# Moving a fused kernel's weights by 64 bytes, and writing the first group's gate into PSUM

## The reference

```python
for t in range(S):                                   # attention
    kt, vt, rt, wt = (k[:, :, t], v[:, :, t], r[:, :, t], w[:, :, t])
    cur = np.einsum('bhd,bhe->bhde', u[None] * kt, vt)
    y[:, :, t] = np.einsum('bhd,bhde->bhe', rt, state + cur)
    state = wt[:, :, :, None] * state + np.einsum('bhd,bhe->bhde', kt, vt)

h = x @ w_in                                         # first network, 384 -> 2048 -> 384
g = np.where(h >= 1, h, np.where(h <= -1, 0.0, (h + 1) ** 2 / 4))
x = g @ w_out

g = x @ w_gate                                       # second network, 384 -> 1536 -> 384
silu = g * (1.0 / (1.0 + np.exp(-g)))
out = silu * (x @ w_val) @ w_out
```

## Time and profile before

| what | value |
|---|---|
| median of 3 runs | 992.36 us (992.11 to 992.6) |
| the profiled execution | 992.52 us |
| its span, first to last instruction | 990.6 us |
| TensorE, VectorE, ScalarE, GpSimd busy | 972.9, 519.5, 402.3, 163.5 us |
| mean granted clock of TensorE | 0.999 of full speed |

### The profile page before, as it was taken

How to read it: one execution, slowest core, us unless ns; L and a number is a source line. 1 busy time by engine, 2 the same in 40 slices (tenths; PEclk the granted TensorE clock), 3 DMA queues, 4 the chain that set the end, 5 groups by cost and what they waited for, 6 DMA issues and landing times.

```text
span 990.6 us, 17480 instructions
## 1 busy us (share of the span) xinstructions
PE 972.9 (98%) x6886; PEld 954.7 (96%) x6886; DVE 519.5 (52%) x906; ACT 402.3 (41%) x841; POOL 163.5 (17%) x155
## 2 busy tenths in 40 slices
PE   6999999999999999999999999999999999999998
PEld 5899999999999999999999999999999999999997
DVE  8996666657576575764444433434333343334332
ACT  5665455454554554544665322222222222222222
POOL 6992210301102112020263200000000000000000
PEclk9999999999999999999999999999999999999999
DMA  9724212121222212100332100010100001010000
GB/s 303 238 66 132 85 55 86 53 86 52 87 77 62 87 43 95 68 2 1 132 108 88 57 17 32 1 49 1 48 0 29 19 0 48 0 48 0 24 1 25
DMA packets 23492, 59.52 MB, mean 60 GB/s; under 512 B 2688, under 2 KB 12032, under 8 KB 23424
## 3 DMA queue, kind: packets, MB, share of 16 engines
q1 hardware_dynamic: 23424, 58.59, 18.2%
HBM read 49.14 MB, written 9.44 MB: 59 GB/s over the span
## 4 chain that ended last, share of the span: by engine, by line
PE 94%; DVE 3%; issue 1%; ACT 1%; DMA 0%; DVEq 0%
PE bank L1202 50%; PE bank L1230 35%; PE bank L1258 2%; PE bank L1280 2%; PE bank L1275 1%; PE bank L1250 1%; DVE suf L965 1%; PE bank L1286 1%; PE bank L1267 1%; DVE att L1031 0%; DVE k_r_by_channel L990 0%; DVE k_r_by_channel L987 0%; DMA w_by_channel<-in_w_channel 0%; DVE glo L1055 0%; DVE gate L1062 0%
## 5 line engine op out<-in xcount | busy, mean ns | idle before, releaser
L806 ACT ACTIVATE ghi<-gate 128x384 fp32r<-128x384 f32 x224 | 117.3, 523 | 186.7 <-DVE gate L1074 95.6
L1055 DVE TENSOR_TENSOR glo<-gate,ghi 128x384 fp32r<-128x384 f32 x224 | 133.7, 597 | 113.2 <-ACT ghi L806 111.0
L1072 DVE TENSOR_TENSOR gate<-bank,gate 128x384 f32<-128x384 f32 x96 | 53.5, 557 | 223.2 <-ACT gate L925 223.2
L1202 PE MATMUL bank<-xhi,w2gv_alo 128*128 128x384 f32 x480 | 162.6, 339 | 0.0
L1202 PE MATMUL bank<-xlo,w2gv_ahi 128*128 128x384 f32 x480 | 162.5, 339 | 0.0
L1202 PE MATMUL bank<-xhi,w2gv_ahi 128*128 128x384 f32 x480 | 162.5, 339 | 0.0
L925 ACT ACTIVATE gate<-bank 128x384 f32<-128x384 f32 x96 | 47.3, 493 | 235.8 <-PE bank L1202 235.8
L1230 PE MATMUL bank<-ghi,w1ohi 128*128 128x384 f32 x384 | 134.8, 351 | 2.0 <-DVE ring L1067 1.1
L1202 PE MATMUL bank<-xhi,w1ihi 128*128 128x384 f32 x384 | 130.3, 339 | 1.3 <-issue 0.8
L1062 DVE SCALAR_TENSOR_TENSOR gate<-bank,gate 128x384 f32<-128x384 f32 x128 | 71.1, 555 | 112.4 <-ACT gate L815 112.4
L1230 PE MATMUL bank<-glo,w1ohi 128*128 128x384 f32 x384 | 130.0, 338 | 0.0
(11 more groups left out here) (95 smaller groups left out, 1580.4 us busy)
## 6 DMA issues: line engine op xcount, KB each, us to landing
r_k_v_by_token<-in_rkv_token SPq DMA_DIRECT2D x24, 576.0 KB, 5.0
k_r_by_channel<-in_kr_channel SPq DMA_DIRECT2D x24, 448.0 KB, 4.0
w_by_channel<-in_w_channel SPq DMA_DIRECT2D x24, 226.2 KB, 2.6
x_t<-ring SPq DMA_DIRECT2D x8, 576.0 KB, 2.8
x_raw<-x_t SPq DMA_DIRECT2D x8, 576.0 KB, 4.0
ring<-in_w_out SPq DMA_DIRECT2D x22, 192.0 KB, 2.5
out_t<-ring SPq DMA_DIRECT2D x7, 576.0 KB, 3.1
ring<-in_w_gate SPq DMA_DIRECT2D x12, 192.0 KB, 2.4
```

The costliest lines, as they stand in the source:

```text
L806: e.activation(ghi[j % 2][:, :], gate[j % 2][:, :], ACT.Copy).then_inc(M["hi", ph], 1)
L1055: e.tensor_tensor(glo[j % 2][:, :], gate[j % 2][:, :], ghi[j % 2][:, :].bitcast(F32), ALU.subtract)\
L1072: e.tensor_tensor(q, hid[j % 2][:, 0:T], q, ALU.mult).then_inc(M["t", 2], 1)
L1202: m = e.matmul(out, w_of(a, k), x_of(b_, k), start=start and i == 0, stop=stop and i == total - 1)
```

## The change

Four things. The three small tiles become one of 80 bytes, placed as 96, and the weights begin at 96 bytes beyond a multiple of 256 from xhi (no padding is needed with the sizes at hand); everything behind them moves down by 64 bytes. In group 0 of the first network the gate goes to the PSUM bank of its product instead of to SBUF: VectorE's knee writes there, and ScalarE's hi and VectorE's lo read it there. For that tile_in waits for lo instead of knee, in group 0 from tile 2 on and for the first two tiles of group 1. And in slot 15 of group 0 VectorE does copy_out before the scan.

```diff
+        xhi_at = at[0]
         xhi = [place(f"xhi{i}", [P, KT, T], F32R)[0] for i in range(2)]
...
-        beyond, _ = place("w_beyond", [PR, 2, OPS_CHECK + 2], F32)
-        bad, _ = place("w_bad", [PR, OPS_CHECK + 1], F32)
-        ones, _ = place("ones", [PR, 9], F32)
-        ones = ones[:, 0:1]
+        sums, _ = place("w_sums", [PR, 3 * OPS_CHECK + 2], F32)
+        beyond = sums[:, 0:2 * OPS_CHECK].rearrange("q (b n) -> q b n", b=2)
+        bad, ones = sums[:, 2 * OPS_CHECK:3 * OPS_CHECK + 1], sums[:, 3 * OPS_CHECK + 1:3 * OPS_CHECK + 2]
+
+        W_STEP = 256
+        at[0] += (xhi_at + 96 - at[0]) % W_STEP
...
-        assert w1_at % 64 == 32
...
+        def gate_of(ph, g, j):
+
+            return hid[j % 2][:, 0:T] if ph == 1 and first(g) else gate[j % 2][:, :]
...
-                e.activation(ghi[j % 2][:, :], gate[j % 2][:, :], ACT.Copy).then_inc(M["hi", ph], 1)
+                e.activation(ghi[j % 2][:, :], gate_of(ph, g, j), ACT.Copy).then_inc(M["hi", ph], 1)
...
-                e.tensor_tensor(glo[j % 2][:, :], gate[j % 2][:, :], ghi[j % 2][:, :].bitcast(F32), ALU.subtract)\
+                e.tensor_tensor(glo[j % 2][:, :], gate_of(ph, g, j), ghi[j % 2][:, :].bitcast(F32), ALU.subtract)\
                     .then_inc(M["lo", ph], 1)
...
-                q = gate[j % 2][:, :]
-                e.scalar_tensor_tensor(q, hid[j % 2][:, 0:T], 1.0, q, ALU.max, ALU.min).then_inc(M["g", 1], 1)
+                e.scalar_tensor_tensor(gate_of(1, g, j), hid[j % 2][:, 0:T], 1.0, gate[j % 2][:, :], ALU.max, ALU.min).then_inc(M["g", 1], 1)
...
+                if j == J1 - 1 and first(g):
+                    copy_out(1, g)
                 if after_next:
                     if j in scan_slots(g):
                         scan_window(g + 2, scan_slots(g)[j])
                 if after_next and j == SUM_SLOT:
                     sum_w(g + 2)
-                if j == J1 - 1:
+                if j == J1 - 1 and not first(g):
                     copy_out(1, g)
...
             def tile_in(g, j, parity):

-                e.wait_ge(M["g", 1], g * J1 + (j - 1) + J1)
+                if first(g) and j > 1 or g == 1 and j < 2:
+                    e.wait_ge(M["lo", 1], g * J1 + (j - 1))
+                else:
+                    e.wait_ge(M["g", 1], g * J1 + (j - 1) + J1)
```

## The result

The changed kernel takes 978.07 us (median of 4 runs, 977.80 to 978.83), the kernel before in the same comparison 992.24 (991.85 to 992.60). The ratio is 0.9859, with a 95% interval of 0.9841 to 0.9876, so it is 14.2 us faster. The forecast was 991.5 us and its range ended at 984.5. The profiled execution has a span of 976.9 us, before 990.6.

A forecast was written before the change was run, and what follows sets the result against it. TensorE's matmul pace and four first-group stops were taken to bound the kernel. +1.1 (wait) - 0.55 (covered stop) - 1.40 (copy), addresses 0, gave -0.85 against the median 992.36: 991.5 us, range 984.5 to 995.7.

The forecast's parts named there:

- What bounds the kernel: TensorE's pace, 4 896 matmuls at 176.7 ns, 865 of 990.6 us, plus four stops in or at the end of the first group.
- The addresses: Weights 64 bytes lower, all matmuls: taken as 0, with bounds of two to four clocks either way, 4.1 to 8.2 us.
- Rival 1: The addresses help every matmul: 987.4 us with two clocks, 983.3 with four; chance 0.28.
- The new wait and the relief: First group: tile_in waits for lo, lo and GpSimd get relief; tile_in(6) +1.1 us, less 0.55 for the covered stop.
- the second gain: First group: GpSimd runs under lo and knee, shortening three VectorE instructions by 0.35 us each, 1.05 us up to lo(4).
- The gain by cover: First group: VectorE's own stop of 0.55 us at 62.5 us is covered by the new delay, -0.55.
- Slots 5 and later: nothing is added: First group: lo(6) ends near 56.2, tile_in(8) starts near 56.3 at its own pace, so no further delay.
- rival 4: The relief doesn't come, since another VectorE instruction then meets GpSimd: 992.6 us; chance 0.15.
- The low part and the knee: First group: glo's subtraction, with one PSUM input, falls from 846 to near 550 ns; the knee stays near 550.
- rival 3: The knee, reading and writing one PSUM bank, takes up to 1.10 us: +2.2 us, 993.7; chance 0.10.
- The copy: Slot 15 of group 0: VectorE's copy before its scan removes TensorE's stop near 101 us, -1.40 us.
- The sum without addresses: New wait +1.1, covered stop -0.55 and earlier copy -1.40 make -0.85 us.

The follow-up runs named there:

- e1: Kernel before with only the three small tiles made one, so all weights stand at 96 instead of 160 bytes; 977.76 us, ratio 0.9854.
- e2: Changed kernel with its weights put back to 160 bytes, leaving gate in PSUM, its waits and the earlier copy; 992.86 us, ratio 1.0004.
- e3: Kernel before with e1's addresses and VectorE's group 0 copy before the scan, gate still in SBUF; 976.17 us, ratio 0.9836.
- e9: e3 with the changed kernel's wait of tile_in for the low part, gate still in SBUF; 978.64 us, ratio 0.9859.
- e5: e4 with x tiles and weights all 64 bytes higher, distances the same; 980.21 us (a single time).
- e8: e3 with all weights at 192 bytes instead of 96; 976.75 us, ratio 0.9852.
- e11: Changed kernel with only the high weights of the second network's tile 5 at 160 bytes; 985.91 us (a single time).
- e12: e8 with only the high weights of the second network's tile 5 at 160 bytes; 976.04 us (a single time).
- e6: Changed kernel with high and low weights of ten second-network tiles at 96 or 160 bytes in different pairings; 982.82 us (a single time).
- e4: Changed kernel with ten second-network gate and value weight tiles each at another distance from xhi modulo 256; 980.17 us (a single time).
- e10: e3 with fewer x columns, x from one address, or repeated x or weight blocks in five second-network tiles; 963.37 us (a single time).
- e13: e3 with 64, 96 and 32 weight columns in three second-network tiles and one repeated column in a fourth; 976.26 us (a single time).

## Why the prediction was wrong

**What bounds the kernel** was right: TensorE's pace, and four stops. So were the two questions, pace and stops, and the count of 4 896 matmuls.

**The addresses** are the step that failed. "I take 0, as for VectorE" rested on a row of another engine, and the bounds of two to four clocks on nothing but caution: no row of before said how many of the 16.7 ns beyond column time could move. Rival 1 (the addresses help, 0.28) named the mechanism, and was sized at 4.1 to 8.2 us. It was eight clocks, 16.3 us by the count, of which 14.7 came through (e1). By the traces of before and e1 that is 8.6 us in the second network; 5.9 in the later groups, where 1 971 matmuls would give 6.6; and 0.4 of 1.1 in group 0, where TensorE waits for VectorE. What the later groups lack lies beside the attention matmuls: the first step of a tile_out behind them stayed at 266 ns, and the step from a tile into them grew by 4. These 14.7 us put the time beyond the range. A bound was to be had from the rows: all 16.7 ns of a matmul, by 4 896, are 82 us, and the steps of before were uneven. In the second network before, neighbouring start times lie 177, 174, 180 and 175 ns apart in turn, so some steps ran 6 ns under others of the same shape. A stream at its shortest step would have taken 174 ns x 4 896, 13 us less. I had taken only the mean. That would have been a hint at the size and no bound, since the pace that came, 173.3 ns, lies below the shortest of these steps.

**The new wait and the relief** had the right sign and less than half the size (+0.55 forecast, +1.45 in e2, 1.9 in the medians). tile_in(2) came 1.13 us later, as forecast (1.1). tile_in(6) came 1.65 later instead of 1.0, because the second gain, which I had taken whole (1.05), was 0.23. The gain by cover, 0.55, came (from +1.76 to +1.21 in e2). "Slots 5 and later: nothing is added" was wrong by 0.24: tile_in(11) waited for lo(9), behind attention work at 71 us. The 1.9 us are the changed kernel less e3. e9 shows the wait bare at 2.5 us in the medians and 3.1 in its trace. The prediction had, without the second gain, 2.15 for it, and 2.5 with the low part of 0.91 left as it was (49.49 plus 0.05 less 47.15, plus 0.1). That this agrees with e9's median is luck: in e9 lo(4) took 0.54 us, and the clock fell. In e2, rival 4 is nearly the case that came (992.6 against 992.86).

**The low part and the knee**: 546 ns near 550 as forecast; the knee 558, so rival 3 (1 100) is false. The lock showed as the row had it, but its second effect didn't: a shorter instruction moves all later turns of the two engines, and what is gained at one is lost at the next (e2). "VectorE and GpSimd are both without a pause there" held for the kernel before only: GpSimd, made faster, ran out of high parts from ScalarE.

**The copy**: -1.40 forecast; in e2 the lead goes from +1.45 to +0.05, -1.40, and in the medians e1 less e3 is 1.6.

**The sum without addresses**: -0.85 forecast, +0.05 in the trace of e2 and +0.4 in the medians, both within 0.2% of before.

**Where the gain of the pace comes from** is settled in part. Shown: it is the distance between weights and the tiles they meet, modulo 256 bytes (e1, e2, e5; 192 bytes gives the same as 96, e8); the stream has at least two rhythms, of 416 and 424 clocks, and carries them on (e11); a tile with its high weights at 160 forces the slow one, 192 returns to the fast (e12), and 96 carries on the slow one behind high weights at 160 alone (e11, e6), not behind every slow tile (e6, e4). Most of the 32 clocks beyond the columns go with reading x at changing addresses (e10) and don't shrink with the width of the weights (e13). Open: why the tiles at 96 do the one or the other, what x's reads meet there, and how the weights' distance enters, when their width doesn't.

## What to carry to other kernels

Where one step is repeated thousands of times, list its start times one by one before taking its mean: an uneven pattern (177, 174, 180, 175 ns) was here the sign of a slower rhythm, and the gap between its mean and its shortest step a first estimate of what an edit without arithmetic can give (13 us; 16.3 by the pace that came). Place weights and streamed tiles at a distance that returned to the fast rhythm (here 192 bytes) rather than one that did not (96), where one tile with its high weights at 160 cost 8.2 us. And when a bank is kept for longer to relieve another engine, price the wait first: here wait and relief together cost 1.9 us, and the best version measured leaves them out (e3, 976.17 us).

## What the runs showed of the hardware that I had not expected

- A move by 64 bytes changes a 384-column matmul from 176.7 to 173.3 ns (e1), and one tile of weights out of place makes 2 475 later matmuls 3.33 ns slower each (e11).
- With x read at one address the same matmul takes 162.5 ns (e10).
- Behind a stop of 2.36 us the granted clock fell to 1.2 GHz for 3.2 us; behind one of 2.06 us, in the changed kernel, it stayed at 2.4.
- A VectorE instruction of 128x384 that reads and writes the same PSUM bank takes 558 ns on average, against 548 in the same stretch of before and 556 in the later groups with its output in SBUF: hardly more.
- The lock between VectorE and GpSimd gave its gain to GpSimd, which then stood for ScalarE: 2.17 us in e2.
